# Attention with two heads side by side in column groups of TensorE, the rotary part of the keys on GpSimd

## The chip, the cores and the metric

The kernel runs on one core of a Trainium2 chip. The metric is the device time of one execution in microseconds. TensorE (PE) multiplies, VectorE (DVE) and ScalarE (ACT) work element by element and can read PSUM, GpSimd (POOL) works on SBUF alone, SyncE (SP) issues the DMAs. Each engine runs its own list of instructions in order; semaphores hold one back until another has done its part.

## The reference

Attention over 4 batches of 8 heads, 576 positions of 64 values, with rotary position encoding of queries and keys, then two feed-forward layers of 512 to 2048 to 512.

```python
q_rot, k_rot = rotate(q), rotate(k)          # x1*cos - x2*sin, x1*sin + x2*cos
scores = 1/sqrt(64) * q_rot @ k_rot.T
scores = scores - max(scores, axis=-1)
attn = exp(scores); attn = attn / (sum(attn) + 1e-09)
x = (attn @ v)                               # to [2304 tokens, 512]
h = x @ w_in;   x = (h - tanh(h)) @ w_out          # layer 1
h = x @ w_in2;  x = (h * sigmoid(1.702*h)) @ w_out2  # layer 2
```

## The kernel before

Attention comes first, then the two layers; the layers (`first_product`, `second_product`, `unit`) are not touched by the change. Numbers that need more than fp32r's precision are kept as a high part and a rest, both fp32r: `k_hl` holds the keys' high part in one half of the partitions and the rest in the other, `q_hh` the queries' high part twice, `q_max` the queries' rest and the rows for the maxima, `k_one` the keys' high part and ones.

32 heads are 16 pairs; the keys of a head are five tiles of 128 (the last of 64). For one head PE does, for each of five tiles:
- near scores M(h, t), line 414: queries by keys, two fp32r matmuls of 288 columns, from which DVE takes the row maxima (`row_max`, line 667);
- after five of them one transpose of the maxima (`maxima_across`, line 421), which DVE copies behind the queries (`place_maxima`, line 674);
- scores S(h, t), lines 431 and 437: keys by queries with the maximum taken off in the product, four fp32r matmuls; ACT makes exp of them (`exp`, line 537, into `probs`, five buffers);
- values, `probs_v`, line 449: two fp32 matmuls of 288 columns. The stationary operand `v_one` is 128 wide: 64 columns of V and 64 of ones, so one product gives both values and sums of a head. PSUM banks 6 and 7 hold the result of one head; ACT copies it out (`copy_pv`, line 545).

The six PSUM banks before are a ring of three slots, used in the order of `RING`, S, M and R (the transpose) alike: PE may write a slot when the use three places back has been read (`slot_free`). The order in a head is S, PV of two tiles back, and M tiles of the next head behind the first two S; it is written out in `ring_order` and again in PE's loop. The transpose stands between the third S and the fourth, so it has two more tiles of its head to cover it.

DVE also does the rotary part, `rope`: three operations of 128x576 for the keys of a pair and three for the queries (lines 659 to 662), one or the other in each head, and the rests (`keys_lo` line 679, `queries_lo` line 684). ACT makes the high parts (`keys_hi`, `queries_hi`). SyncE loads, makes the second copies in `k_one` and `q_hh` by DMA, and carries the sums: from `pv_sb` to `sums`, inverted by DVE (`invert`), through DRAM to all partitions (`inv_wide`). GpSimd multiplies (`normalise`, line 382, two operations of 64x576 a pair) and SyncE stores the result. In heads 17 to 31 the x chunks and weights of the first layer are split ahead of time (`early_x`, `early_w`), in DVE's and ACT's lists.

## Time and profile before

| what | us |
|---|---|
| runs | 1146.66, 1146.83, 1147.7; median 1146.83 |
| the profiled execution | 1147.27 |
| its span, first to last instruction | 1145.5 |
| PE busy | 1104.1 (96%) |
| DVE busy | 552.4 (48%) |
| ACT busy | 425.7 (37%) |
| POOL busy | 57.1 (5%) |

TensorE's granted clock is 0.997 of 2.4 GHz over the span. Busy time of PE counts records that overlap: a record of a matmul lasts longer than it takes the next one to start, since the pipeline is long, so the pace is read from the starts. A fp32 matmul of the program is two records with a weight load each; a fp32r one is one record. The shares are means over attention and the layers, which have different limits.

### The profile page before, as it was taken

To read this page: it belongs to the slowest core of one execution; us is meant where nothing else is said; L and a number is where in the kernel's file an instruction comes from. 1 tells how busy PE (TensorE), PEld (TensorE's weight loads), DVE (VectorE), ACT (ScalarE), POOL (GpSimd) and SP (SyncE) were. 2 spreads that over 40 slices of the span, in tenths; PEclk is the share of its full clock that TensorE was granted. 3 is DMA by queue.
4 is the path that set the end of the run, shared out by engine and by line. 5 is a ranking of instruction groups with operands and counts; after the bars stand their busy time and mean duration, and the time that the engine had idled before them with its cause. 6 is when DMAs were issued, how large, how long until landed. Compare 5 with 4: busy or idle time off the path is not lost.

```text
span 1145.5 us, 15078 instructions
## 1 busy us (share of the span) xinstructions
PE 1104.1 (96%) x5952; PEld 1017.8 (89%) x5952; DVE 552.4 (48%) x879; ACT 425.7 (37%) x747; POOL 57.1 (5%) x62
## 2 busy tenths in 40 slices
PE   2999998999999999999999999999999999999998
PEld 1888877787789999999999999999999999999997
DVE  7888887888736433232233333455232322323222
ACT  2555554555544423222222323445232222323222
POOL 3011111102111000000000000000000000000000
PEclk9999999999999999999999999999999999999999
DMA  6355557566315300000000100062000000000000
GB/s 182 95 158 127 155 154 201 136 169 166 87 61 178 102 28 29 28 28 11 19 28 28 29 28 28 1 193 83 28 28 28 28 1 28 28 28 1 28 1 28
DMA packets 78854, 79.85 MB, mean 70 GB/s; under 512 B 30144, under 2 KB 55744, under 8 KB 78784
## 3 DMA queue, kind: packets, MB, share of 16 engines
q1 hardware_dynamic: 78784, 78.89, 24.1%
q8 instruction: 47, 0.77, 0.3%
q14 instruction: 23, 0.19, 0.1%
HBM read 55.12 MB, written 14.23 MB: 61 GB/s over the span
## 4 chain that ended last, share of the span: by engine, by line
PE 89%; DVE 7%; SPq 1%; DMA 1%; POOL 1%; issue 1%; ACT 0%; POOLq 0%; DVEq 0%; ACTq 0%
PE PS L485 35%; PE PS L503 17%; PE PS L500 17%; PE PS L449 10%; PE PS L414 3%; PE PS L431 3%; PE PS L437 3%; DVE neg_max L667 2%; DVE q_max L684 1%; DVE k_hl L679 1%; DVE q_max L674 1%; DMA turned_k<-k_dram 1%; DVE raw_q L662 0%; DVE w_parts L697 0%; DVE raw_q L660 0%
## 5 line engine op out<-in xcount | busy, mean ns | idle before, releaser
L485 PE MATMUL PS<-x_hi,w_parts 128*128 128x384 f32 x1536 | 423.1, 336 | 0.0
L742 DVE TENSOR_TENSOR g_raw<-PS,act_t 128x384 f32<-128x384 f32 x192 | 107.0, 557 | 400.2 <-ACT act_t L610 202.1
L485 PEld LDWEIGHTS PS<-x_hi,w_parts 128*128 128x128 f32 x1536 | 280.5, 188 | 4.3
L485 PE MATMUL PS<-x_lo,w_parts 128*128 128x384 f32 x768 | 257.2, 335 | 0.0
L500 PE MATMUL PS<-g_hi,w_parts 128*128 128x384 f32 x768 | 210.3, 334 | 0.8 <-DVE g_lo L747 0.8
L503 PE MATMUL PS<-w_parts,g_hi 128*128 128x512 f32 x576 | 195.1, 393 | 1.0 <-DVE y_sb L756 0.8
L449 PE MATMUL PS<-probs,v_one 128*128 128x288 f32 x640 | 183.4, 409 | 0.3 <-ACT pv_sb L545 0.3
L747 DVE TENSOR_TENSOR g_lo<-g_raw,g_hi 128x384 fp32r<-128x384 f32 x192 | 107.7, 561 | 113.6 <-ACT g_hi L617 113.6
L537 ACT ACTIVATE probs<-PS 128x576 f32<-128x576 f32 x160 | 104.0, 650 | 129.6 <-PE PS L437 126.3
L485 PEld LDWEIGHTS PS<-x_lo,w_parts 128*128 128x128 f32 x768 | 144.2, 188 | 4.2
L617 ACT ACTIVATE g_hi<-g_raw 128x384 fp32r<-128x384 f32 x192 | 100.8, 525 | 122.9 <-DVE g_raw L742 119.7
L500 PEld LDWEIGHTS PS<-g_hi,w_parts 128*128 128x128 f32 x768 | 140.0, 188 | 1.1 <-DVE g_lo L747 1.1
L449 PEld LDWEIGHTS PS<-probs,v_one 128*128 128x128 f32 x640 | 112.4, 191 | 18.1 <-issue 0.5
L667 DVE TENSOR_REDUCE neg_max<-PS 128x1 f32<-128x576 f32 x160 | 113.8, 746 | 30.1 <-PE PS L414 29.5
L500 PE MATMUL PS<-g_lo,w_parts 128*128 128x384 f32 x384 | 128.3, 334 | 0.0
L503 PEld LDWEIGHTS PS<-w_parts,g_hi 128*128 128x128 f32 x576 | 108.1, 188 | 21.9 <-issue 1.1
L610 ACT ACTIVATE act_t<-PS 128x384 f32<-128x384 f32 x96 | 47.2, 492 | 212.5 <-PE PS L485 212.5
L608 ACT ACTIVATE act_t<-PS 128x384 f32<-128x384 f32 x96 | 47.2, 492 | 206.9 <-PE PS L485 206.9
L414 PE MATMUL PS<-k_hl,q_hh 128*128 128x288 f32 x320 | 86.7, 376 | 34.8 <-DMA q_hh<-q_hh 17.5
L503 PE MATMUL PS<-w_parts,g_lo 128*128 128x512 f32 x288 | 113.7, 395 | 0.0
L414 PEld LDWEIGHTS PS<-k_hl,q_hh 128*128 128x128 f32 x320 | 56.4, 200 | 51.8 <-issue 19.7
L431 PE MATMUL PS<-q_hh,k_hl 128*128 128x288 f32 x320 | 80.0, 332 | 0.0
(51 smaller groups left out, 741.3 us busy)
## 6 DMA issues: line engine op xcount, KB each, us to landing
x_raw<-x_scratch SPq DMA_DIRECT2D x12, 768.0 KB, 4.5
raw_w<-moe_w_in_dram SPq DMA_DIRECT2D x32, 256.0 KB, 3.1
raw_w<-moe_w_out_dram SPq DMA_DIRECT2D x32, 256.0 KB, 3.3
raw_k<-k_dram SPq DMA_DIRECT2D x16, 288.0 KB, 3.5
turned_k<-k_dram SPq DMA_DIRECT2D x64, 72.0 KB, 3.2
raw_q<-q_dram SPq DMA_DIRECT2D x16, 288.0 KB, 3.8
turned_q<-q_dram SPq DMA_DIRECT2D x64, 72.0 KB, 3.5
k_one<-k_hl SPq DMA_DIRECT2D x32, 144.0 KB, 2.4
```

Source lines behind the costliest of these rows:

```text
L414: last = nc.tensor.matmul(slot[:, b, :], q_hh[h % 4][:, t * P:(t + 1) * P], k_hl[h % 4][:, b * HALF:(b + 1) * HALF], start=True, stop=True)
L431: nc.tensor.matmul(slot[:, b, :], k_hl[h % 4][:, keys], q_hh[h % 4][:, b * HALF:(b + 1) * HALF], start=True, stop=False)
L449: last = nc.tensor.matmul(pv_banks[:, b, :], v_one[h // 2 % 2][:, h % 2, t, :], probs[g % PROBS][:, b * HALF:(b + 1) * HALF], start=t == 0 ...
L485: last = nc.tensor.matmul(h_banks[j % 2], w_parts[j][:, w, c * P:(c + 1) * P], x[par][:, c, :], start=(c == 0 and w == 0 and x is x_hi), s ...
L500: last = nc.tensor.matmul(acc_banks[c][:, 0:UNIT], w_parts[j][:, w, c * P:(c + 1) * P], g[:, s, :], start=start, stop=stop)
L503: last = nc.tensor.matmul(acc_banks[c], g[:, s, c * P:(c + 1) * P], w_parts[j][:, w, :], start=start, stop=stop)
L537: nc.scalar.activation(probs[g % PROBS][:, :].rearrange("p (b n) -> p b n", b=2), slot_halves(slot_of("S", h, t)), ACT.Exp).then_inc(exp_d ...
L608: nc.scalar.activation(act_t[:, j % 2, :], h_banks[j % 2], ACT.Tanh).then_inc(act_done, 1)
L617: nc.scalar.activation(g_hi[:, j % STAGES, :], g_raw[:, j % 2, :], ACT.Copy).then_inc(g_hi_done, 1)
L667: nc.vector.tensor_reduce(neg_max[h % 2][:, t:t + 1], slot_halves(slot_of("M", h, t)), AX.XY, ALU.max, negate=True).then_inc(max_done, 1)
L742: nc.vector.tensor_tensor(g_raw[:, j % 2, :], h_banks[j % 2], act_t[:, j % 2, :], ALU.subtract if m == 0 else ALU.mult).then_inc(g_done, 1)
L747: nc.vector.tensor_tensor(g_lo[:, j % STAGES, :], g_raw[:, j % 2, :], g_hi[:, j % STAGES, :].bitcast(F32), ALU.subtract).then_inc(g_lo_don ...
```

## The change

The loops go by pairs, and each step does tile n of both heads.

- `values(unit)` replaces `probs_v`. V of both heads lies in one tile, `v_sb` (laid out so by the host's `value_tiles`); head 0's 64 columns of it go to columns 0 to 63 of the array and PSUM partitions 0 to 63, head 1's to the other half, in matmuls of 512 and of 64 columns. The sums are four matmuls of 288 columns by 32 ones, one for each half of each head, in four groups of 32 columns. Eight fp32 matmuls (sixteen records) replace four (eight).
- `copy_pv` is once a pair: three copies of 512, 64 and 288 columns. The result is one tile of 128x576, normalised in place in one GpSimd operation.
- The rotary part of the keys from pair 1 on is three GpSimd operations a pair; DVE keeps the queries, and both of pair 0.
- The maxima of a pair go out together: two transposes in one slot, in the last step, and the order of M tiles follows `near_plan`. Before the first S all ten M tiles of pair 0 are done.
- Six sets of `k_hl`, `k_one`, `q_hh`, `q_max` instead of four, six `probs` instead of five, some of them in memory that the layers use later.
- The early weights and x stand in pairs 8 to 15.

In the diff the first `rope` is GpSimd's, the last loop over pairs is DVE's, and `split` is `keys_lo` and `queries_lo` of one head.

```diff
+def near_plan(pair):
+    if pair == 0:
+        return [(0, 0), (0, 2), (2, 2), (2, 2), (0, 0)]
+    return [(1, 2), (1, 2), (1, 1), (1, 1), (0, 0)]
...
+        values_wide, values_tail, sum_rows = PS[:, 6, :], PS[:, 7, 0:TAIL], PS[:, 7, TAIL:TAIL + HALF]
...
-            for j in range(4):
+            for j in range(SETS):
                 nc.gpsimd.memset(k_one[j][:, :].bitcast(F32), 0.0)
...
+            def rope(pair):
+                par = pair % 2
+                pool.wait_ge(loaded["k"][par], (pair // 2 + 1) * 80)
+                nc.gpsimd.tensor_tensor(turned["k"][par][:, :], turned["k"][par][:, :], sin_sb[:, :], ALU.mult).then_inc(pool_chain, 1)
+                nc.gpsimd.tensor_tensor(raw["k"][par][:, :], raw["k"][par][:, :], cos_sb[:, :], ALU.mult).then_inc(pool_chain, 1)
+                pool.wait_ge(pool_chain, 3 + 2 * pair)
+                nc.gpsimd.tensor_tensor(raw["k"][par][:, :], raw["k"][par][:, :], turned["k"][par][:, :],
+                                        ALU.add).then_inc(k_roped, 1)
...
+            for pair in range(PAIRS):
                 if pair >= 2:
+                    normalise(pair - 2)
+                if pair + 3 < PAIRS:
+                    rope(pair + 3)
...
-            def probs_v(g):
-                h, t = divmod(g, TILES)
-                pe.wait_ge(exp_done, g + 1)
+            def values(unit):
+                pair, t = divmod(unit, TILES)
+                pe.wait_ge(exp_done, 2 * unit + 2)
                 if t == 0:
-                    pe.wait_ge(loaded["v"][h // 2 % 2], h // 4 * 64 + 64)
-                    if h:
-                        pe.wait_ge(pv_copied, h)
-                for b in range(2):
-                    last = nc.tensor.matmul(pv_banks[:, b, :], v_one[h // 2 % 2][:, h % 2, t, :],
-                                            probs[g % PROBS][:, b * HALF:(b + 1) * HALF], start=t == 0, stop=t == TILES - 1)
-                last.then_inc(pv_done, 1)
+                    pe.wait_ge(loaded["v"][pair % 2], pair // 2 * 16 + 16)
+                    if pair:
+                        pe.wait_ge(pv_copied, pair)
+                first, last = t == 0, t == TILES - 1
+                p = [probs[(2 * unit + a) % PROBS] for a in range(2)]
+                for bank, cols in ((values_wide, slice(0, BANK)), (values_tail, slice(BANK, SEQ))):
+                    for a in range(2):
+                        nc.tensor.matmul(bank[own(a), :], v_sb[pair % 2][:, t, own(a)], p[a][:, cols],
+                                         start=first, stop=last, skip_group_check=True)
+                for g in range(4):
+                    done = nc.tensor.matmul(sum_rows[32 * g:32 * g + 32, :], ones[:, t // FULL, :],
+                                            p[g // 2][:, g % 2 * HALF:(g % 2 + 1) * HALF], start=False, stop=last,
+                                            skip_group_check=True)
+                done.then_inc(pv_done, 1)
...
+            for h, t in near_tiles(0):
+                near_scores(h, t)
+            maxima_across(0)
+            for pair in range(PAIRS):
+                for n, (first, second) in enumerate(pair_steps(pair)):
+                    scores(2 * pair, n)
+                    for h, t in first:
+                        near_scores(h, t)
+                    if pair * TILES + n:
+                        values(pair * TILES + n - 1)
+                    if n == TILES - 1 and pair + 1 < PAIRS:
+                        maxima_across(pair + 1)
+                    scores(2 * pair + 1, n)
+                    for h, t in second:
+                        near_scores(h, t)
...
+            def copy_pv(pair):
+                act.wait_ge(pv_done, (pair + 1) * TILES)
+                if pair >= 3:
+                    act.wait_ge(x_stored[(pair - 3) % 2], (pair - 3) // 2 * 16 + 16)
+                nc.scalar.activation(pv_sb[pair % 3][:, 0:BANK], values_wide, ACT.Copy)
+                nc.scalar.activation(pv_sb[pair % 3][:, BANK:SEQ], values_tail, ACT.Copy)
+                if pair >= 2:
+                    act.wait_ge(sums_in[pair % 2], pair // 2 * 64)
+                nc.scalar.activation(sum_sb[pair % 2][:, :], sum_rows, ACT.Copy).then_inc(pv_copied, 1)
...
+            for pair in range(PAIRS):
+                a, b = 2 * pair + 4, 2 * pair + 5
+                for n, (first, second) in enumerate(pair_steps(pair)):
...
+                    for h, t in first + second:
+                        row_max(h, t)
+                    if pair and b < NHEADS and n == 1:
+                        split(a)
+                    if pair and b < NHEADS and n == 3:
+                        split(b)
+                    if n == 3 and pair:
+                        invert(pair - 1)
+                    if n == TILES - 1 and pair + 1 < PAIRS:
+                        for h in (2 * pair + 2, 2 * pair + 3):
+                            place_maxima(h)
...
+                    if n == TILES - 1 and pair + 3 < PAIRS:
+                        rope(pair + 3)
```

PE's list in the first half of a head in the steady part, before. L431 and L437 are S, L449 is PV of one head, L414 is M of the next head.

```order
L431 MATMUL PS<-q_hh,k_hl 128x288 x2
L437 MATMUL PS<-q_max,k_one 128x288 x2
L449 MATMUL PS<-probs,v_one 128x288 x2
L414 MATMUL PS<-k_hl,q_hh 128x288 x4
L431 MATMUL PS<-q_hh,k_hl 128x288 x2
L437 MATMUL PS<-q_max,k_one 128x288 x2
L449 MATMUL PS<-probs,v_one 128x288 x2
L421 MATMUL PS<-ident,neg_max 5x128
L431 MATMUL PS<-q_hh,k_hl 128x288 x2
```

PE's list in one step of a pair and the start of the next, now. L466 and L472 are S, L447 is M, L488 the values of both heads, L492 the four sums.

```order
L466 MATMUL PS<-q_hh,k_hl 128x288 x2
L472 MATMUL PS<-q_max,k_one 128x288 x2
L447 MATMUL PS<-k_hl,q_hh 128x288 x2
L488 MATMUL PS<-probs,v_sb 64x512 x2
L488 MATMUL PS<-probs,v_sb 64x64 x2
L492 MATMUL PS<-probs,ones 32x288 x4
L466 MATMUL PS<-q_hh,k_hl 128x288 x2
L472 MATMUL PS<-q_max,k_one 128x288 x2
L447 MATMUL PS<-k_hl,q_hh 128x288 x4
L466 MATMUL PS<-q_hh,k_hl 128x288 x2
L472 MATMUL PS<-q_max,k_one 128x288 x2
L447 MATMUL PS<-k_hl,q_hh 128x288 x2
```

The work on values stands in one block a step, between the two heads' scores, instead of one behind each S.

DVE's list for one head before (L667 is a row maximum, L659 to L662 the rotary part, L674 the placing of the maxima, L679 and L684 the rests):

```order
L667 TENSOR_REDUCE neg_max<-PS 128x1 x5
L659 TENSOR_TENSOR turned_k<-turned_k,sin_sb 128x576
L660 TENSOR_TENSOR raw_k<-raw_k,cos_sb 128x576
L662 TENSOR_TENSOR raw_k<-raw_k,turned_k 128x576
L674 TENSOR_TENSOR q_max<-PS,g_raw 5x640
L679 TENSOR_TENSOR k_hl<-raw_k,k_hl 64x576
L684 SCALAR_TENSOR_TENSOR q_max<-raw_q,q_hh 64x576
```

DVE's list for one pair now (L743 is a row maximum, L755 and L760 the rests, L767 and L769 the inverse, L750 the placing, L736 to L739 the rotary part of the queries):

```order
L743 TENSOR_REDUCE neg_max<-PS 128x1 x6
L755 TENSOR_TENSOR k_hl<-raw_k,k_hl 64x576
L760 SCALAR_TENSOR_TENSOR q_max<-raw_q,q_hh 64x576
L743 TENSOR_REDUCE neg_max<-PS 128x1 x4
L755 TENSOR_TENSOR k_hl<-raw_k,k_hl 64x576
L760 SCALAR_TENSOR_TENSOR q_max<-raw_q,q_hh 64x576
L767 TENSOR_SCALAR sums<-sums 128x9
L769 RECIPROCAL sums<-sums 128x9
L750 TENSOR_TENSOR q_max<-PS,g_raw 5x640 x2
L736 TENSOR_TENSOR turned_q<-turned_q,sin_sb 128x576
L737 TENSOR_TENSOR raw_q<-raw_q,cos_sb 128x576
L739 TENSOR_TENSOR raw_q<-raw_q,turned_q 128x576
```

Both placings stand together at the end of a pair, behind the rests of the second head, with the rotary part behind them; three operations of the keys are gone.

## Rows read from the trace of the kernel before

**Rows 1.** The page: span, and busy time of each engine (share) xinstructions
```profile
span 1145.5 us, 15078 instructions
...
PE 1104.1 (96%) x5952; PEld 1017.8 (89%) x5952; DVE 552.4 (48%) x879; ACT 425.7 (37%) x747; POOL 57.1 (5%) x62
```

**Rows 2.** Sums by stretch: length, busy time by engine, clock, DMA share, GB/s
```profile
100.90:119.10 18.20, 18.16 (x105) 15.51 (x104) 16.00 (x25) 10.44 (x17) 2.81 (x2) 1.00 0.57 149
155.50:319.60 164.10, 151.16 (x819) 126.59 (x818) 136.60 (x194) 86.91 (x135) 26.91 (x18) 0.98 0.56 147
319.60:340.30 20.70, 20.39 (x112) 17.54 (x110) 5.94 (x9) 8.65 (x13) 4.21 (x3) 1.00 0.17 55
340.30:1145.50 805.20, 800.11 (x4309) 761.11 (x4307) 279.00 (x480) 252.59 (x481) 3.07 (x2) 1.00 0.12 39
```

**Rows 3.** Timeline, first scores of pairs 0, 2, 15: start, us, engine, line
```profile
23.82 0.68 PE L431 MATMUL PS<-q_hh,k_hl 128*128 128x288 f32 x2
...
64.50 0.42 PE L431 MATMUL PS<-q_hh,k_hl 128*128 128x288 f32 x2
...
319.57 0.42 PE L431 MATMUL PS<-q_hh,k_hl 128*128 128x288 f32 x2
```

**Rows 4.** Timeline of PE in a steady pair, its PV groups
```profile
114.75 1.15 PE L449 MATMUL PS<-probs,v_one 128*128 128x288 f32 x4
...
116.37 1.13 PE L449 MATMUL PS<-probs,v_one 128*128 128x288 f32 x4
...
117.86 1.13 PE L449 MATMUL PS<-probs,v_one 128*128 128x288 f32 x4
...
119.62 1.13 PE L449 MATMUL PS<-probs,v_one 128*128 128x288 f32 x4
```

**Rows 5.** Timeline, scores handed to ScalarE
```profile
200.46 0.43 PE L437 MATMUL PS<-q_max,k_one 69*128 69x288 f32 x2
...
200.93 0.65 ACT L537 ACTIVATE probs<-PS 128x576 f32<-128x576 f32 x1 [0.55 <-PE PS L437]
```

**Rows 6.** Timeline, ScalarE copies and makes exp, GpSimd beside, PE after
```profile
331.46 0.65 ACT L545 ACTIVATE pv_sb<-PS 128x576 f32<-128x576 f32 x1 [0.32 <-PE PS L449]
...
331.85 1.40 POOL L382 TENSOR_TENSOR x_out<-pv_sb,inv_wide 64x576 f32<-64x576 f32 x1 [10.84 <-DMA inv_wide<-inv_scratch]
332.01 0.65 ACT L537 ACTIVATE probs<-PS 128x576 f32<-128x576 f32 x1
...
332.26 0.72 PE L449 MATMUL PS<-probs,v_one 128*128 128x288 f32 x2 [0.31 <-ACT pv_sb L545]
```

**Rows 7.** Instructions by line and form: busy us, mean ns of one, idle before
```profile
L667 DVE TENSOR_REDUCE neg_max<-PS 128x1 f32<-128x576 f32 x160 | 113.8, 746 | 30.1 <-PE PS L414 29.5
...
L537 ACT ACTIVATE probs<-PS 128x576 f32<-128x576 f32 x160 | 104.0, 650 | 129.6 <-PE PS L437 126.3
...
L382 POOL TENSOR_TENSOR x_out<-pv_sb,inv_wide 64x576 f32<-64x576 f32 x32 | 48.3, 1508 | 298.0 <-DMA inv_wide<-inv_scratch 246.4 <-issue 50.7
...
L674 DVE TENSOR_TENSOR q_max<-PS,g_raw 5x640 fp32r<-5x640 f32 x32 | 25.9, 811 | 2.9 <-PE PS L421 2.5
...
L625 ACT ACTIVATE y_sb<-PS 128x512 f32<-128x512 f32 x10 | 5.4, 596 | 2.2 <-PE PS L503 2.2
L625 ACT ACTIVATE y_sb<-PS 128x384 f32<-128x384 f32 x12 | 5.2, 488 | 2.2 <-PE PS L500 2.2
```

**Rows 8.** Timeline, a split of VectorE beside GpSimd's product
```profile
185.80 1.68 POOL L382 TENSOR_TENSOR x_out<-pv_sb,inv_wide 64x576 f32<-64x576 f32 x1 [21.05 <-issue]
186.24 1.87 DVE L684 SCALAR_TENSOR_TENSOR q_max<-raw_q,q_hh 64x576 fp32r<-64x576 f32 x1
```

**Rows 9.** Timeline of the start: GpSimd's fourth set, VectorE's first rotary operation
```profile
8.07 0.14 POOL L369 MEMSET q_hh<- 128x64 f32 x1
...
9.90 0.70 DVE L659 TENSOR_TENSOR turned_k<-turned_k,sin_sb 128x576 f32<-128x576 f32 x1
```

**Rows 10.** Who waited for whom on PE in attention: us, times, longest
```profile
PE PS L414 <- DVE neg_max L667: 12.6, 9, 3.1
```

420 lines of the change are left out of this document (218 added, 202 removed).

## The prediction, made before the changed kernel ran

> **What bounds the kernel now.** I read the page's busy times first, then the sums by stretch, then one pair of heads in the timeline, then the waits. The page shows TensorE (PE) busy for 96% of 1145.5 us [rows 1]. The stretches say which part the change can touch: from 340.3 us on PE only runs the two layers, whose code is the same in both kernels, so 805 us are fixed. Attention, 0 to 340 us, has four pieces [rows 2, 3]: a start up to the first scores of pair 2 (64.5 us); five steady pairs, 18.2 us each, with PE busy 18.16 of 18.20 us in the one shown; eight pairs from 155.5 to 319.6 us, 20.5 us each, with PE busy 151 of 164 us; and a last pair of 20.7 us, of which 2.1 us are twelve fp32r matmuls of the first layer (384 columns at the pace of 0.27 us for two of 288, below), so 18.6 us are attention. In the eight slow pairs PE's near scores wait for row maxima, 12.6 us over all of attention [rows 10]: VectorE (DVE) has the weight and x splits of the early layer in its queue there, and it is busy 16.0 of 18.2 us even in a steady pair [rows 2].
>
> The pair in parts [rows 4]. From one PV group to the next is 1.49 us where scores alone stand between them (116.37 to 117.86); two fp32r matmuls (one near-score tile, M) add 0.27 (117.86 to 119.62); the transpose of the maxima adds 0.13 (114.75 to 116.37). A fp32 matmul is two records, each with a weight load of its own; four records last 1.13 us and the last of them 0.41, so one pass of 288 columns takes (1.13 - 0.41) / 3 = 0.24 us, and one head's PV tile four passes = 0.96. A score tile (S) is then 1.49 - 0.96 = 0.53. A pair is 10 S + 10 M + 2 transposes + 10 PV = 5.3 + 2.7 + 0.26 + 9.6 = 17.9 us of the 18.2: PE is the bound, with 0.3 us of waiting.
>
> **What the change does to PE.** One call of `values` replaces two PV tiles. By columns, a pass of 512 is 0.24 x 512 / 288 = 0.43 us and one of 64 is 0.05. If the column groups work beside each other, the unit costs 2 x 0.43 (both heads' first 512 columns) + 2 x 0.05 + 2 x 0.24 (the four sums) = 1.44; I take 1.5 for sixteen starts instead of eight. The pair falls to 5.3 + 2.7 + 0.26 + 5 x 1.5 = 15.8 us of PE work, 2.1 less. No row of the kernel before has a matmul with fewer than 128 columns of weights, but for the transpose, so the bounds of a unit are 1.44 below and, above, all sixteen passes in a row: 4 x 0.43 + 4 x 0.05 + 8 x 0.24 = 3.84, twice the 1.92 of now. I take the lower end because the 0.24 is the streaming of columns and the groups stream apart.
>
> **New waits.** PE's order is new, and it runs in order through a ring of three slots; a wait there delays all that follows. Handing over costs 0.20 us from the end of streaming to ScalarE (ACT): the record of the last scores ends at 200.89, 0.16 after its stream, and exp starts at 200.93 [rows 5]. Back to PE it costs 0.15 (ACT's copy ends 332.11, PE's row starts 332.26 [rows 6]). With exp 0.65, row maximum 0.74, place 0.81 [rows 7] and the fact that DVE starts an operation about 0.07 before the last one's record ends, one pair has:
> - The maxima of both heads go out together. The first of the two transposes to the first `place_maxima` done and back is 0.20 + 0.81 + 0.15 = 1.16; PE has the second transpose, S of the second head and half an S meanwhile, 0.13 + 0.53 + 0.27 = 0.93. Wait 0.25 to 0.3.
> - The next pair's first M takes the slot of the transposes and waits for the second place, 0.74 later, with 0.27 of scores to cover it: 0.45.
> - M tiles of step 0 wait for the first row maximum, queued behind three rotary operations of the queries (3 x 0.70 [rows 9]): 0.25.
> - Step 1's first S takes the slot of the second head's S of step 0. Its exp stands behind `copy_pv`, now three copies. Copies of 512 and 384 columns take 0.596 and 0.488 [rows 7], so 64 takes 0.22 and 288 takes 0.41; each starts 0.1 before the last ends (332.01 against 332.11 [rows 6]), 0.9 in all. From the end of `values`: 0.20 + 0.9 + 0.65 + 0.15 = 1.9, against S + 2 M + the wait above = 1.3 on PE: 0.6.
> - Step 2's first S waits for the exp of the second head's S of step 1: 0.20 + 0.65 + 0.15 = 1.0 against 2 M = 0.53: 0.45.
> - Step 3's first S waits for a row maximum that stands behind the splits of the next head (`split(a)`): 0.2, and 0.8 when a split collides with GpSimd (below).
> - The last unit waits for the exp just before it: 1.0 - 0.27 - 0.53 = 0.2.
>
> That is 2.4 to 3.1 us. The new pair is 15.8 + 2.4 = 18.2, to 15.8 + 3.1 = 18.9; I take 18.6. So the 2.1 us won on PE are given back as waits at handovers, because PE's work between them has become shorter while the exp, maxima and copies have not.
>
> **Rotary part on GpSimd.** It takes three operations of 128x576 per pair from DVE (2.1 us of DVE's 16.0) and gives them to GpSimd, where one of 64x576 costs 1.51 mean, 1.4 alone [rows 6, 7]; more lanes at the same column count should cost the same. GpSimd goes from 2 operations to 4 a pair, 2.8 to 5.6 us. When a DVE operation with two operands in SBUF meets one of these it stands until it is through: the split at 186.24 takes 1.87 instead of 0.75, ending 0.6 after GpSimd's operation of 185.80 does [rows 8]. Row maxima, which read PSUM, are not held. GpSimd's block of four (5.6 us, from inv_wide's arrival on) meets `split(a)` in most pairs; none met costs 0, one met up to 1.4 on DVE, of which 0.6 reaches PE by the item above. The Trainium skill (SBUF — State Buffer, "SBUF: two separate sides") calls the shared port pair an exclusive lock, held for the whole instruction; the trace agrees with its 1.87 us.
>
> **Start.** GpSimd clears six sets, not four: four sets end at 8.21 [rows 9], having begun at 2.88, so two more at 1.33 us each end at 10.9, while the clears of v_one behind them go. DVE's first rotary operation moves from 9.90 [rows 9] to 11.3. Before the first S there are ten row maxima instead of five (+3.4 us), and the splits of the second head ahead of them (+1.5), less the 3 rotary operations of keys that stood there (-2.2): first S near 27 against 23.8, near 30 if GpSimd's keys of pair 1 meet DVE's first rotary operations. Pairs 0 and 1 then run by DVE's list (9 rotary operations, 12 splits, 20 maxima, 4 places: 6.3 + 8.4 + 13.5 + 3.0 = 31 us, and some 10 us of waiting for first exps and copies), about 41.5 us against 40.7. Pair 2 starts at 68 to 73; I take 70.
>
> **The slow pairs.** DVE's list is three operations shorter, so a weight split (two per head pair at most) fits: DVE has 13.9 + 1.2 = 15.1, with a collision 16.5, of 18.6. I leave no dent there. This is the only place of real gain.
>
> **Sum** against the profiled execution (1147.3 us, its span 1145.5 and 1.8 around it): start 70 - 64.5 = +5.5; thirteen pairs 13 x 18.6 = 241.8 against 319.6 - 64.5 = 255.1, -13.3; last pair 5.3 + 7.5 + waits where no M covers (5 or so of about 1 us) = 18.1 against 18.6, -0.5. Together -8.3: 1139.0. The median of the runs is 0.4 below the profiled execution, so 1138.6, and I say 1139. SyncE issues about as many DMAs a pair as before (23 against 24) and hides them; at the end of attention the inverse of the last pair has several units to travel, as before.
>
> **Rivals.**
> 1. *The waits are shorter than laid out.* For: the ring may run further ahead than my handovers allow. Then a pair is 15.8 + 0.9 = 16.7, thirteen are 38 us shorter, start +3.5, last pair -2: -36.5, 1110 us. Against: seven handovers of 0.2 and more are all in the rows.
> 2. *The array drains when the column tiling changes.* A record outlasts its streaming by 0.41 - 0.24 = 0.16 us [rows 4]; three changes a unit (whole array to halves to quarters and back) make it 1.5 + 0.48 = 1.98. Eighty units are 38 us, of which about 6 are waits that PE has anyway: 1139 + 32 = 1171 us. The transpose, the one narrow matmul of now, shows no such cost (0.13 us for 128 columns). The Trainium skill (TensorEngine Tiling (Array Packing), "Tiling Modes") says that changing the mode drains the engine; no run here shows it yet.
> 3. *The other side, in one mechanism: passes start strictly in order.* In `values` both passes of one matmul stand together. The second waits for the first on the same columns, and the other head's first pass behind it. Then only neighbours overlap: 3 x 0.43 + 2 x 0.05 + 5 x 0.24 = about 2.55 a unit, 1.05 more; 80 x 1.05 = 84, of which about 19 cover waits that PE has anyway (row maxima and splits have more time): 1139 + 65 = 1204 us. For: PE's records start in order everywhere. It decides as soon as a unit is over 1.6 us, since each 0.1 us is 8 us of kernel. The Trainium skill (TensorE: Matmul & The Clock Gate, "Part 3: Packing small matmuls — row/col tiling") has matmuls in strict order in start and end; that would give this case.
> 4. *The groups don't overlap at all.* 3.84 a unit, 80 x 2.34 = 187 less the same 19: 1139 + 168 = 1307 us. The change doesn't do what it says then.
>
> **Chances.** Forecast (overlap and waits as laid out, 1126 to 1150) 0.50; rival 1 0.18; rival 2 0.13; rival 3 0.11; rival 4 0.06; 0.02 for others. A run of this kernel can be told from no change at about 0.2%, 2.3 us. Faster: 0.18 + 0.50 x 0.72 = 0.54. Same: 0.08. Slower: 0.06 of the forecast's own tail and rivals 2 to 4 and the rest: 0.38. The range 1104 to 1185 takes in the forecast, rival 2 and most of rival 1, and leaves out 3 and 4 and the far end of 1, just under 0.2.
>
> **What would show it.** Right: from one unit of `values` to its end 1.5 us; starts of two column groups together; pairs of 18.2 to 18.9 us with PE's idle time at the first S of steps 1, 2 and 3 and behind q_max; rotary operations on GpSimd with DVE splits of 1.5 to 2.2 us beside them; pair 2 at about 70 us; the layers as long as before. Wrong: a unit of over 1.6 us (rivals 2 to 4), a pair under 17.5 (rival 1), or pairs 8 to 15 longer than pairs 2 to 7.

## The result, and the profile after

The changed kernel takes 1188.24 us (median of 4 runs, 1183.38 to 1191.1), the kernel before 1146.74 beside it: ratio 1.0356, 95% interval 1.032 to 1.0392. It is 3.6% slower, 49 us above the forecast. The profiled execution took 1187.16 us.

The page of the kernel after (compare [rows 1]); parts 1, 2 and 4:

```profile
span 1185.4 us, 16265 instructions
PE 1118.9 (94%) x6592; PEld 953.3 (80%) x6592; DVE 540.2 (46%) x835; ACT 418.1 (35%) x763; POOL 109.0 (9%) x93
PEclk9899999999999999999999999999999999999999
PE 82%; DVE 13%; ACT 2%; issue 2%; POOL 1%; DMA 1%; SPq 0%; POOLq 0%; DVEq 0%; ACTq 0%
```

PE is still most of the chain that ended last. Its busy sum is 15 us above that of [rows 1] although fewer columns are streamed, and the span grew by 40. The stretches say where. They are cut at the first scores of pairs 0, 2, 7 and 15 (length, busy time by engine, granted clock, DMA share, GB/s):

```profile
0.00:31.06 31.06, 6.34 (x22) 4.54 (x23) 20.89 (x29) 4.10 (x6) 19.26 (x38) 0.99 0.59 163
31.06:77.74 46.68, 41.15 (x271) 24.67 (x269) 34.22 (x48) 20.80 (x34) 8.40 (x6) 0.89 0.39 103
77.74:183.63 105.89, 95.41 (x712) 57.87 (x711) 77.79 (x106) 49.63 (x85) 33.10 (x20) 1.00 0.50 129
183.63:357.82 174.19, 155.70 (x1139) 93.62 (x1137) 126.11 (x170) 81.98 (x140) 43.32 (x26) 0.98 0.50 137
357.82:1185.40 827.58, 820.28 (x4458) 772.58 (x4456) 281.23 (x485) 261.57 (x498) 4.93 (x3) 1.00 0.12 40
```

Against [rows 2, 3]: up to pair 2 77.7 us for 64.5 (+13.2); five pairs 105.9 for 91.0 (+14.9); eight pairs 174.2 for 164.1 (+10.1); from pair 15 to the end 827.6 for 825.9 (+1.7). That is the 39.9.

**One unit of values.** PE, and below it PE's weight loads, of one unit in pair 4 (L447 M, L488 the values, L492 the sums, L466 the next S):

```profile
122.28 0.53 PE L447 MATMUL PS<-g_hi,g_lo 128*128 128x288 f32 x2 [0.25 <-DVE q_max L750]
122.74 0.64 PE L488 MATMUL PS<-probs,v_sb 128*64 128x512 f32 x1
122.74 0.64 PE L488 MATMUL PS<-y_sb,v_sb 128*64 128x512 f32 x1
123.22 0.59 PE L488 MATMUL PS<-probs,v_sb 128*64 128x512 f32 x1
123.22 0.59 PE L488 MATMUL PS<-y_sb,v_sb 128*64 128x512 f32 x1
123.64 0.22 PE L488 MATMUL PS<-probs,v_sb 128*64 128x64 f32 x1
123.65 0.22 PE L488 MATMUL PS<-y_sb,v_sb 128*64 128x64 f32 x1
...
123.86 0.44 PE L492 MATMUL PS<-probs,ones 128*32 128x288 f32 x2
123.87 0.44 PE L492 MATMUL PS<-y_sb,ones 128*32 128x288 f32 x2
124.13 0.41 PE L492 MATMUL PS<-probs,ones 128*32 128x288 f32 x2
...
124.48 0.53 PE L466 MATMUL PS<-q_hh,k_hl 128*128 128x288 f32 x2
```
```profile
122.73 0.13 PEld L488 LDWEIGHTS PS<-probs,v_sb 128*64 128x64 f32 x1 [0.16 <-ACT y_sb L580]
...
124.48 0.30 PEld L466 LDWEIGHTS PS<-q_hh,k_hl 128*128 128x128 f32 x2 [0.47 <-issue]
```

The two heads start together (122.74), their second passes together (123.22), the four sums together (123.86): the column groups overlap wholly. The gaps are elsewhere. A record ends 0.16 after its stream, so M's streaming ends at 122.28 + 0.53 - 0.16 = 122.65; the first weights of the tiled matmuls go in at 122.73 and their stream starts at about 122.79 (the second pass at 123.22 less its 0.43), 0.14 later. The tails' stream ends at 123.76 and the sums start at about 123.88: 0.12. The sums' second pass streams to 124.38, and only at 124.48 does the weight load of the next S begin (between matmuls of the whole array it lies under the streaming before it), so S streams from about 124.58: 0.20. Three changes of tiling, 0.46 us a unit on top of 1.48 of streaming. The starts of streams are worked out from rows and good to some 0.02 us.

The whole unit from rows of pair 5, where nothing is waited for:

```profile
156.90 1.19 PE L488 MATMUL PS<-probs,v_sb 128*64 128x512 f32 x8
158.03 0.69 PE L492 MATMUL PS<-probs,ones 128*32 128x288 f32 x8
158.65 0.53 PE L466 MATMUL PS<-g_lo,g_hi 128*128 128x288 f32 x2
...
160.19 0.64 PE L488 MATMUL PS<-probs,v_sb 128*64 128x512 f32 x1
```

From unit to unit 3.29 us, with two S and one M between (2 x 0.53 + 0.27 = 1.33): a unit is 1.96 us. Two PV tiles before were 1.92 [rows 4]. The quarter of the columns that the change saves is spent on the changes of tiling.

**The waits.** PE in pair 5, its rows with idle time ahead of them (in brackets):

```profile
142.55 0.50 PE L472 MATMUL PS<-q_max,k_one 69*128 69x288 f32 x2 [0.41 <-DVE q_max L750]
143.30 0.53 PE L447 MATMUL PS<-k_hl,q_hh 128*128 128x288 f32 x2 [0.25 <-DVE q_max L750]
...
147.26 0.53 PE L466 MATMUL PS<-g_lo,g_hi 128*128 128x288 f32 x2 [0.42 <-ACT y_sb L580]
...
151.53 0.54 PE L466 MATMUL PS<-g_lo,g_hi 128*128 128x288 f32 x2 [0.21 <-ACT y_sb L580]
...
155.91 0.53 PE L466 MATMUL PS<-g_lo,g_hi 128*128 128x288 f32 x2 [0.58 <-DVE neg_max L743]
```

These are five of the seven places that the prediction lists, with the releasers it names. The brackets miss the 0.16 by which a record outlasts its stream; with it the five are 2.7 us. For the other two places no row shows idle time. The pair lasts 21.0 us and its work is 5.3 + 2.7 + 0.26 + 5 x 1.96 = 18.1, so 2.9 us are waits. The last of the five is the collision. VectorE, then GpSimd, in front of it:

```profile
153.33 1.85 DVE L760 SCALAR_TENSOR_TENSOR q_max<-raw_q,q_hh 64x576 fp32r<-64x576 f32 x1
155.11 1.40 DVE L743 TENSOR_REDUCE neg_max<-PS 128x1 f32<-128x576 f32 x2
```
```profile
152.64 1.93 POOL L401 TENSOR_TENSOR turned_k<-turned_k,sin_sb 128x576 f32<-128x576 f32 x1
154.54 1.92 POOL L402 TENSOR_TENSOR raw_k<-raw_k,cos_sb 128x576 f32<-128x576 f32 x1
156.54 1.41 POOL L404 TENSOR_TENSOR raw_k<-raw_k,turned_k 128x576 f32<-128x576 f32 x1
```

Alone a 128x576 operation takes 1.41 us on GpSimd, as 64x576 did. When they meet, both records get longer (1.93 and 1.85), and the ends show that they take turns: GpSimd's first ends at 154.57, VectorE's split 0.61 later (155.18), GpSimd's second 1.28 after that (156.46). Each stands until the other's operation is through.

**The start.** VectorE's rotary part of the first queries, and beside it GpSimd's of pair 1:

```profile
13.55 1.96 DVE L728 TENSOR_TENSOR turned_q<-turned_q,sin_sb 128x576 f32<-128x576 f32 x1
15.43 1.95 DVE L729 TENSOR_TENSOR raw_q<-raw_q,cos_sb 128x576 f32<-128x576 f32 x1
17.41 1.83 DVE L731 TENSOR_TENSOR raw_q<-raw_q,turned_q 128x576 f32<-128x576 f32 x1
```
```profile
13.42 1.47 POOL L401 TENSOR_TENSOR turned_k<-turned_k,sin_sb 128x576 f32<-128x576 f32 x1 [2.56 <-DMA turned_k<-k_dram]
14.86 1.91 POOL L402 TENSOR_TENSOR raw_k<-raw_k,cos_sb 128x576 f32<-128x576 f32 x1
16.84 1.79 POOL L404 TENSOR_TENSOR raw_k<-raw_k,turned_k 128x576 f32<-128x576 f32 x1
```

VectorE's three take 5.7 us, 3.5 more than at 0.75, and all that follows stands behind them: first M at 22.5, first S at 31.1.

**The clock.** The mean granted clock was 1.00 in eleven of the pairs from 2 to 14 and 0.93 in pairs 8 and 10, so for a part of those two at the lower of its two levels, 1.2 GHz. Those two took 23.6 and 23.4 us from first exponential to first exponential; the other six of pairs 7 to 14 took 21.1 on average, as much as a steady pair. The kernel before has two such pairs too, 8 and 14, with 24.4 and 22.4 us.

### The profile page after: what moved, and what is told of

Same layout as the page of the kernel before. It is cut to its first block, busy times and chain, and to the rows that moved or that the text cites. A ratio compares the mean times of both kernels' runs of the same rounds, so it can differ in the third digit from the quotient of the medians.

```text
span 1185.4 us, 16265 instructions
## 1 busy us (share of the span) xinstructions
PE 1118.9 (94%) x6592; PEld 953.3 (80%) x6592; DVE 540.2 (46%) x835; ACT 418.1 (35%) x763; POOL 109.0 (9%) x93
## 4 chain that ended last, share of the span: by engine, by line
PE 82%; DVE 13%; ACT 2%; issue 2%; POOL 1%; DMA 1%; SPq 0%; POOLq 0%; DVEq 0%; ACTq 0%
PE PS L529 33%; PE PS L547 17%; PE PS L544 17%; PE PS L488 5%; DVE neg_max L743 4%; PE PS L492 3%; PE PS L466 3%; DVE q_max L760 3%; PE PS L447 2%; DVE q_max L750 2%; PE PS L472 2%; DVE k_hl L755 1%; ACT y_sb L580 1%; DVE g_hi L755 1%; ACT probs L580 0%
## 5 line engine op out<-in xcount | busy, mean ns | idle before, releaser
L743 DVE TENSOR_REDUCE neg_max<-PS 128x1 f32<-128x576 f32 x160 | 116.0, 752 | 82.2 <-PE PS L447 82.0
L580 ACT ACTIVATE y_sb<-PS 128x576 f32<-128x576 f32 x79 | 51.4, 652 | 90.7 <-PE PS L472 90.4
L580 ACT ACTIVATE probs<-PS 128x576 f32<-128x576 f32 x81 | 52.5, 650 | 71.2 <-PE PS L472 70.9
L472 PE MATMUL PS<-q_max,k_one 69*128 69x288 f32 (+1 forms) x320 | 70.4, 302 | 5.9 <-DVE q_max L750 5.7
L447 PE MATMUL PS<-k_hl,q_hh 128*128 128x288 f32 x220 | 47.8, 317 | 28.3 <-DMA q_hh<-q_hh 22.9
L544 PEld LDWEIGHTS PS<-g_lo,w_parts 128*128 128x128 f32 x384 | 72.1, 188 | 0.0
L488 PE MATMUL PS<-probs,v_sb 128*64 128x512 f32 (+1 forms) x324 | 67.9, 438 | 0.8 <-ACT probs L580 0.6
```

Source lines behind the costliest of these rows:

```text
L447: last = nc.tensor.matmul(slot[:, b, :], q_hh[h % SETS][:, t * P:(t + 1) * P], k_hl[h % SETS][:, b * HALF:(b + 1) * HALF], start=True, sto ...
L472: last = nc.tensor.matmul(slot[:, b, :], k_one[h % SETS][rows, keys], q_max[h % SETS][rows, b * HALF:(b + 1) * HALF], start=False, stop=True)
L488: nc.tensor.matmul(bank[own(a), :], v_sb[pair % 2][:, t, own(a)], p[a][:, cols], start=first, stop=last, skip_group_check=True)
L544: last = nc.tensor.matmul(acc_banks[c][:, 0:UNIT], w_parts[j][:, w, c * P:(c + 1) * P], g[:, s, :], start=start, stop=stop)
L580: nc.scalar.activation(probs[i % PROBS].rearrange("p (b n) -> p b n", b=2), slot_halves(slot_of("S", h, t)), ACT.Exp).then_inc(exp_done, 1)
L743: nc.vector.tensor_reduce(neg_max[h % 2][:, t:t + 1], slot_halves(slot_of("M", h, t)), AX.XY, ALU.max, negate=True).then_inc(max_done, 1)
```

## The experiments

Three theories, of which more than one can hold. A: the changes of tiling eat what the columns save. B: PE's new order of work waits more. C: GpSimd's rotary part blocks VectorE. (The expectations of single runs have letters of their own; their ranges are called first, second and third below.) Pair starts are read at the first exponential of a pair. Every kernel in a row, in us (the time is the median, the parts are of the profiled execution; the last column has the pairs of 2 to 14 whose mean granted clock was below 0.99):

| kernel | time | to pair 2 | pairs 2 to 6 | pairs 7 to 14 | lower clock |
|---|---|---|---|---|---|
| before | 1146.7 to 1148.4 | 65.2 | 91.0 | 164.1 | 8, 14 |
| changed | 1188.2 | 79.1 | 105.9 | 173.9 | 8, 10 |
| whole-array values | 1191.6 | 79.2 | 109.7 | 174.2 | 12 |
| four changes a unit | 1195.5 | 80.2 | 109.6 | 173.5 | none |
| sums in the last unit only | 1170.5 | 77.9 | 105.5 | 161.1 | 2, 3, 8, 9, 14 |
| keys on VectorE | 1207.9 | 84.6 | 112.5 | 184.3 | 3, 5, 6, 8, 10 to 13 |
| before, PV in two groups | 1178.7 | 71.3 | 105.7 | 171.6 | none |
| before, keys on GpSimd | 1174.2 | 72.4 | 96.3 | 172.9 | 8, 13 |
| two units together | 1167.9 | 89.1 | 96.6 | 159.2 | none |
| other places of M | 1177.0 | 80.0 | 102.3 | 167.4 | 7 |
| two units, start anew | 1160.6 | 76.7 | 96.8 | 159.9 | none |
| copies behind, in addition | 1156.8 | 73.2 | 98.0 | 159.9 | none |
| start anew alone | 1185.8 | 76.2 | 110.1 | 171.8 | 2 |
| start again | 1156.2 | 69.0 | 98.4 | 160.8 | none |

The last column is needed to read the others: a pair at the lower clock is longer by its clock alone (in "keys on VectorE" below, by 1.5 us).

### Whole-array values in the changed kernel

```diff
-(the two loops of values and the four sums)
+for a in range(2):
+    for b in range(2):
+        matmul(wide[b], v_sb[pair % 2][:, t, :], p[a][:, b * HALF:(b + 1) * HALF], ...)
```

> The values and sums of a unit are replaced by four fp32 matmuls of 288 columns on the whole array (128 columns of weights), as in the kernel before: V of both heads as the weights for each head's exp, sums left out, the result is not attention's. Everything else (order, copies, GpSimd's rotary part, waits) is the changed kernel. Theory A (the tiled unit costs 1.94 us with three drains of 0.12 to 0.20 at changes of tiling, just what 1.92 us of whole-array matmuls cost; the 40 us come from the new order's waits and start): 1183 to 1191 us, no change against the changed kernel. Theory B (narrow matmuls are what costs the time): falls to about 1150 us.

Measured: 1191.58 us (1188.91 to 1192.54), ratio 1.0376 (1.0359 to 1.0394). With no tiling at all and the old columns, the time is within 4 us of the changed kernel, 0.6 above the first range and far from the second one's 1150. A tiled unit is worth as much as an untiled one; and the 40 us are still there, so they belong to the order and the start.

### A fourth change of tiling

```diff
-values wide, values tail, sums
+values tail, sums, values wide
```

> Same matmuls, other order inside a unit: the 64-column tail of both heads, then the four sums, then the 512 columns of both heads. The tiling changes four times a unit (whole, halves, quarters, halves, whole) instead of three. Theory A (a change drains the array, 0.12 to 0.20 us by the trace): +0.12 to 0.2 us on 80 units, 10 to 16 us, so 1197 to 1204 us. Theory C (the gaps in the trace come from waits or exposed weight loads at the group's ends and not from changes of tiling): 1186 to 1190 us.

Measured: 1195.48 (1192.26 to 1198.18), ratio 1.0413 (1.0389 to 1.0437). 7 us for 80 more changes, 0.09 each: between the two ranges, in the direction of the first. By itself this shows little, since pairs 2 to 6 also take 109.7 and 110.1 us in two kernels that have no more changes than the changed one (the table); that part of a change falls into waits is a reading, not shown.

### Sums only in the last unit of a pair

```diff
-for g in range(4):
+for g in range(4) if last else ():
```

> The four sum matmuls run only in the last unit of a pair (left out: the sums over the first four key tiles). In 64 of 80 units 0.48 us of streaming and one change (0.12) go. Theory A (PE's work and its waits are in one chain): 64 x 0.6 = 38 us less, of which waits fill a part: 1150 to 1162 us. Theory D (VectorE's list or handovers are the bound in attention and PE merely waits): under 10 us less, 1178 to 1187.

Measured: 1170.51 (1169.1 to 1177.63), ratio 1.0214 (1.0176 to 1.0252), 18 us less, between the two ranges. What leaves PE is 64 times a sum (0.48) and a change (0.12), 38 us. Half of it turned into waits. Pairs 2, 3 and 5 (the last three numbers of a row: granted clock, DMA share, GB/s):

```profile
77.90:99.80 21.90, 18.12 (x110) 11.77 (x110) 15.98 (x22) 9.92 (x17) 6.58 (x4) 0.92 0.45 124
99.80:123.30 23.50, 19.68 (x111) 12.38 (x110) 16.25 (x22) 10.02 (x17) 6.47 (x4) 0.85 0.45 116
143.10:163.50 20.40, 16.58 (x110) 10.93 (x110) 16.02 (x22) 9.91 (x17) 6.59 (x4) 1.00 0.49 133
```

The five together take 105.5 for 105.9, but pairs 2 and 3 ran partly at the lower clock. Pairs 4 to 6, at full clock in both kernels, take 60.0 us for 62.9: 2.9 less of the 7.2 that left PE. The rest are longer waits at the same places. In pair 5 PE stands 1.92 us where it stood 0.58, and 1.04 where it stood 0.41:

```profile
156.02 0.52 PE L466 MATMUL PS<-g_lo,g_hi 128*128 128x288 f32 x2 [1.92 <-DVE neg_max L743]
163.00 0.50 PE L472 MATMUL PS<-q_max,k_one 69*128 69x288 f32 x2 [1.04 <-DVE q_max L750]
```

That is B: the pair is set in part by the chain from scores over row maxima and placed maxima back to PE, and not by PE's work alone. It is also the forecast's own case. The five units of a pair are here 4 x 1.36 + 1.96 = 7.4 us, 1.5 each, as forecast, and the pair takes 20.0 us at full clock, not 18.6.

### Keys' rotary part back on VectorE

```diff
-nc.gpsimd.tensor_tensor(...)   # three a pair
+nc.vector.tensor_tensor(...)   # ahead of those of the queries
```

> The rotary part of all keys goes back to VectorE, directly ahead of that of the queries; GpSimd only normalises. Theory A (the order of PE's work and what it waits for is the loss, GpSimd's lock a minor part): VectorE gets 2.1 us a pair more in the place where the first row maximum of a pair waits for it, loses 1 to 2 us of blocked splits: 1180 to 1200 us. Theory E (GpSimd's operations blocking VectorE are the loss): falls by 20 us or more, 1150 to 1165.

Measured: 1207.93 (1207.43 to 1209.77), ratio 1.0525 (1.051 to 1.0541): 20 us slower and above both ranges. C falls as the main cause: without the collisions a pair at full clock is no shorter (21.6 us for 21.4). In this order VectorE does its rotary part right behind the placed maxima, and the first row maxima of a pair stand behind it. PE's waits for row maxima show it (us, times, longest; changed kernel first):

```profile
PE PS L466 <- DVE neg_max L743: 11.3, 11, 1.7
```
```profile
PE PS L441 <- DVE neg_max L738: 27.7, 14, 4.0
```

Part of the 20 us is the clock. Of pairs 2 to 10 the four at full clock took 21.6 us each, against 21.4 for the same four in the changed kernel, and the five at 0.93 took 23.1. PE falls to half its pace behind the 1.66 us that it stands for a row maximum (a record of 0.64 before is 1.12 here):

```profile
156.04 0.53 PE L441 MATMUL PS<-k_hl,q_hh 128*128 128x288 f32 x2 [1.66 <-DVE neg_max L738]
157.53 1.12 PE L482 MATMUL PS<-probs,v_sb 128*64 128x512 f32 x1
```

Pair 4 has the same wait and stays at 1.00, so not each such wait brings it. What the six operations cost by their place alone is therefore less than the 20 us, and no run gives it at one clock.

### The kernel before, its PV in two column groups

```diff
 for b in range(2):
-    matmul(pv_banks[:, b, :], v_one[..., t, :], probs[...])
+    for a in range(2):
+        matmul(pv_banks[own(a), b, :], v_one[..., t, own(a)], probs[...])
```

> The kernel before, with one edit: each values matmul of a head (128 stationary columns, 288 moving columns) is issued as two, one for each half of its stationary columns, side by side in two column groups of 64. Same operands, same output, same order, same everything else; only the tiling of the array changes, twice in each of the 160 head-units (from whole to two groups before values, and back after). Theory A (the array drains at every change of tiling: 0.14 us into it and 0.20 us out of it in the trace of the changed kernel, and the matmul stream is what bounds the kernel before): 160 x 0.34 = 54 us more, less what falls into waits that are there anyway in the slow pairs: 1185 to 1202. Theory B (a change of tiling costs nothing, and the changed kernel's time went to its order of work alone): within 5 us of the kernel before, 1142 to 1152. Theory C (only the weight loads of the tiled matmuls stand still, some 0.07 a change): 1160 to 1172.

Measured: 1178.67 (1177.44 to 1178.73), ratio 1.026 (1.0244 to 1.0275). 30.5 us slower with the same columns, order and results. The sum over one steady pair ([rows 2] have it at 18.20 us, PE 18.16, 105 PE rows):

```profile
113.60:134.70 21.10, 21.10 (x144) 13.11 (x146) 16.12 (x25) 10.43 (x16) 2.82 (x2) 1.00 0.48 127
```

2.9 us for ten PV tiles with two changes each: 0.145 us a change where PE is the bound. It is not the doubled number of matmuls: the eight records of a tile last 1.19 us together, 0.06 more than the four before (1.13 [rows 4]), and the other 0.23 of the 0.29 lies at the two edges. In pairs 7 to 14, which have waits, only 7.5 of 23 us come through (some 3 more, by estimate, if the two pairs of the kernel before at the lower clock are set aside), and so the total is under the 54 of the first range. The time lies in none of the three ranges; B alone (no more than 5 us) is out: a change of tiling costs by itself.

### The kernel before, keys' rotary part on GpSimd

```diff
-rope("kq"[h % 2], h // 2 + 2)        # VectorE
+if h % 2: rope("q", h // 2 + 2)      # VectorE
+rope(pair + 2)                       # GpSimd, keys, ahead of normalise
```

> The kernel before, with one part of the change: from the second pair on GpSimd does the rotary part of the keys (three operations of 128x576 a pair), VectorE that of the queries alone. If VectorE's row maxima are what the eight slow pairs of the kernel before wait for, taking 2.2 us of it a pair away gives back part of the 18.5 us by which these pairs are longer than 18.2 each: 1133 to 1145. If the collision of GpSimd and VectorE (1.8 us for an operation of 0.75) falls on row maxima and splits of the tight pairs, it costs up to 1 us a pair: 1147 to 1160; and the start is longer by 2 to 5 us in either case, since GpSimd's first rotary part lies beside VectorE's. I take 1144.

Measured: 1174.17 (1168.58 to 1180.98), ratio 1.0226 (1.0183 to 1.0269). I had expected 1144, and it is above the other range too. VectorE, then GpSimd, in a steady pair:

```profile
129.69 1.77 DVE L704 SCALAR_TENSOR_TENSOR q_max<-raw_q,q_hh 64x576 fp32r<-64x576 f32 x1
```
```profile
129.03 1.82 POOL L391 TENSOR_TENSOR turned_k<-turned_k,sin_sb 128x576 f32<-128x576 f32 x1 [11.10 <-DMA turned_k<-k_dram]
```

The keys' operations now meet VectorE's splits, and the row maximum behind them comes 0.8 us late: 19.3 us a pair for 18.2. PE's waits for row maxima rise from 12.6 us [rows 10] to 27.5. So the collision alone is worth 1.1 us a pair where nothing else waits, and C holds as a part: to move work to GpSimd costs here about half of what it frees on VectorE. Of the profiled execution's excess 7.2 us are in the start, 5.3 in pairs 2 to 6 and 8.8 in pairs 7 to 14. It is the fastest of the four; the others took 1173.58, 1174.75 and 1180.98 us at a mean clock of 0.991, 0.990 and 0.988 for its 0.995.

### Two units of values together

```diff
-values(pair * TILES + n - 1)                       # every step
+if n == 0: values([prev]);  if n in (2, 4): values([two units])
-    return [(1, 2), (1, 2), (1, 1), (1, 1), (0, 0)]
+    return [(2, 1), (1, 1), (2, 1), (1, 1), (0, 0)]
```

> The changed kernel, with values of two units back to back (wide and tail of both, then the sums of both) at the third and the fifth step of a pair, so that a pair has 9 changes of tiling in place of 15, and 3, 2, 3, 2 of the next pair's near scores in its steps (2 and 1, 1 and 1, 2 and 1, 1 and 1). Theory A (a change costs 0.12 to 0.20 us, 6 fewer a pair): 0.9 us less a pair, 14 in all, and with fewer waits at steps without values up to 1 us a pair more: 1160 to 1175. If the waits take it all back: 1183 to 1192. If the steps without values starve the matmul stream: above 1195.

Measured: 1167.91 (1167.1 to 1171.08), ratio 1.0174 (1.0154 to 1.0194), 20 us less. A double unit:

```profile
134.59 1.19 PE L488 MATMUL PS<-y_sb,v_sb 128*64 128x512 f32 x8
...
136.69 0.69 PE L495 MATMUL PS<-y_sb,ones 128*32 128x288 f32 x8
...
137.79 0.53 PE L466 MATMUL PS<-q_hh,k_hl 128*128 128x288 f32 x2
```

3.20 us from its first row to the first of S, against 1.74 for a single one (122.74 to 124.48); with the 0.2 that lies outside these rows 3.4 against 3.9. Two doubles a pair save 1.0. A pair fell from 21.0 to 19.2, and the other 0.8 us are waits that the new places of M took away. Pairs 0 and 1 became 10 us longer: without values in their first steps PE stands longer for the copies of the next heads, which come late there (12.1 us of waits from 31 us to pair 2, for 7.3). Beside it the clock was lower for longer (some 21 us after 36 us, for some 5), and the two are not told apart.

### Only other places of M

```diff
-    return [(1, 2), (1, 2), (1, 1), (1, 1), (0, 0)]
+    return [(0, 1), (2, 1), (2, 1), (2, 1), (0, 0)]
```

> The changed kernel, with only the places of the next pair's near scores changed: none in the first step before the unit of values and one behind it, then two before and one behind in the three steps that follow. Theory A (half of the loss is waits of the order, not work): the order of the near scores alone moves the time: at the pair's start the first unit of values no longer stands behind a near score that waits for the second head's placed maxima, 0.5 to 1 us less a pair: 1172 to 1181. If the waits only move: 1185 to 1191. If three near scores in a step are more than VectorE's row maxima keep up with: 1195 to 1205.

Measured: 1176.96 (1174.56 to 1178.31), ratio 1.0242 (1.0219 to 1.0264). The same instructions, in another order of ten of PE's near scores a pair, give 11 us, inside the first range: B is shown by itself.

### The start laid out anew, with the double units and alone

```diff
+pool.wait_ge(q_lo_done, 2)            # ahead of GpSimd's first rope
-for j in range(SETS): (pads)          # VectorE, ahead of the first rope
+set_pads((0, 1)); rope_first(k, q); set_pads((2, 3, 4, 5))
+rope(1)                               # VectorE, ahead of the first row maxima
```

> Both together: values of two units back to back with that run's places of the near scores, and the start laid out anew: GpSimd's first rotary part waits until VectorE has split the first pair's heads, two of the six sets of padding are set before the first rotary part, VectorE rotates the queries of the second pair before the first row maxima and those of the third pair in the first pair's second step, ScalarE makes the high parts of the first four heads before the first exponential. If the 13.2 us which the start costs over the kernel before are such waits, and a matmul stream at half clock behind them, the two effects add: 15 to 22 us less than 1167.9, 1146 to 1153. If the stream fills the start anyway (the half clock of the first 20 us stays, whatever waits are gone): 1159 to 1165.

Measured: 1160.59 (1159.6 to 1163.26), ratio 1.0111 (1.0091 to 1.013). This lies in the second range.

> The changed kernel with the start laid out anew alone (as in the first run of this list), its pairs as they were. The start is 77.7 us to the third pair in the changed kernel and 64.5 in the kernel before. If the order of the first 60 us is what costs it: 7 to 12 us less than 1188.2, 1176 to 1181. If it is the unit of values and the waits of the pairs that also fill the first two pairs: 2 to 5 us less, 1183 to 1186.

Measured: 1185.77 (1184.59 to 1187.98), ratio 1.0327 (1.0304 to 1.0351). Alone it brings 2.4 us, in the second range, but the runs of the two kernels overlap (1183.4 to 1191.1 against 1184.6 to 1188.0), so that is not told from nothing. In the trace 2.9 go up to pair 2, and then pairs 2 to 6 are 4.2 longer, of which 2.2 are pair 2 at a clock of 0.93, and pairs 7 to 14 are 2.1 shorter. With the double units it brings 7, mostly what those had lost in pairs 0 and 1. Pads and GpSimd's first block were only moved onto VectorE's next operations there (in the trace of the next kernel, whose start is the same, two operations of rope(1) take 1.97 and 1.84 us, and PE waits 3.8 us for a row maximum).

### Copies behind both exponentials, and the start once more

```diff
 exp(2 * pair, n)
-if n == 0 and pair: copy_pv(pair - 1)
 exp(2 * pair + 1, n)
+if n == 0 and pair: copy_pv(pair - 1)
...
-    return [(2, 1), (1, 1), (2, 1), (1, 1), (0, 0)]
+    return [(2, 2), (0, 1), (2, 1), (1, 1), (0, 0)]
```

> The kernel of the run before in this list, with ScalarE's copies of the sums of products (1.2 us a pair) behind both first exponentials of a pair in place of between them, and 4, 1, 3, 2 near scores in a pair's steps in place of 3, 2, 3, 2. If the score that waits 0.2 us for an exponential behind the copies is what is left of the waits of a pair: 0.2 to 0.4 us less a pair, 3 to 5 us less. If the two waits of 0.2 us that the trace shows in a pair only move: within 2 us of that run.

Measured: 1156.8 (1155.83 to 1159.23), ratio 1.0077 (1.0058 to 1.0096). 3.8 us less as forecast, but from the time up to pair 2 (3.5), not from the steady pairs (98.0 for 96.8): the number was right and its reason wrong. In those two pairs the clock went down twice in the run before it (at 47 and 61 us) and here not again once it was up, so the 3.5 can be the clock.

```diff
-pool.wait_ge(q_lo_done, 2)
+pool.wait_ge(q_roped, 1)              # GpSimd's first rope, later
-set_pads((2, 3, 4, 5))                # VectorE
+for j in range(2, SETS): nc.gpsimd.memset(k_one[j][max_rows(j % 2), 0:SEQ], 1.0)
...
-    return [(2, 2), (0, 1), (2, 1), (1, 1), (0, 0)]
+    return [(2, 1), (1, 1), (2, 1), (1, 1), (0, 0)]
```

> The kernel with the copies behind both exponentials, with three more edits: GpSimd sets the padding of the last four pairs' sets itself while it is idle (2.8 us of VectorE ahead of the first splits go), GpSimd's first rotary part waits until VectorE has rotated the queries of the second pair (two operations of 1.97 and 1.84 us in place of 0.75, and a wait of 3.8 us of the matmul stream behind them), and 3, 2, 3, 2 near scores in a pair's steps in place of 4, 1, 3, 2 (19.2 us a pair in place of 19.5). Start 3 to 4 us less, five pairs up to 1 us less: 1151 to 1154, still above the kernel before. If the collision in the start only moves to the first row maxima and splits: 1155 to 1158. Below 1146.7 only if the start ends as early as that of the kernel before.

Measured: 1156.21 (1154.38 to 1160.01), ratio 1.008 (1.0061 to 1.0099). VectorE, then GpSimd, in its start:

```profile
16.13 0.75 DVE L743 TENSOR_TENSOR raw_q<-raw_q,cos_sb 128x576 f32<-128x576 f32 x1
```
```profile
17.92 1.40 POOL L408 TENSOR_TENSOR turned_k<-turned_k,sin_sb 128x576 f32<-128x576 f32 x1 [4.57 <-DVE raw_q L745]
```

No operation is stretched, and the first exponential comes at 28.1 us for 27.1 before. The profiled executions differ by 2.9 us, the medians by 0.6: the step is there in the trace and not to be told in the times. The time lies in the second range, though its reason, a collision that only moves, did not come. This order is still 0.8% behind the kernel before. Its pairs take 19.2 to 19.8 us for 18.2; no version tried beats it.

## Why the prediction was wrong

Two steps failed. Both are in the sum for a pair, 15.8 us of work and 2.4 to 3.1 of waits.

- **The unit of `values`, "I take 1.5 for sixteen starts instead of eight".** It measured 1.96. I read from the transpose that a narrow matmul costs nothing extra; but the transpose (128x5) has few columns of weights and does not split the array into groups, so its 0.13 us [rows 4] said nothing on that. The overlap was right, and rivals 3 and 4 are out: the first passes of both heads start at one time, and the second passes too. Rival 2 had the mechanism and the size (1.98). The Trainium skill (TensorEngine Tiling (Array Packing), "Tiling Modes") says that a change of mode drains the engine; by this trace it is 0.12 to 0.20 us, and 0.145 in the kernel before with two groups.
- **The waits as a term that is added to whatever PE does.** The number was right, 2.9 us for 2.4 to 3.1, and so were five of the seven places; that it fits is luck in part, for it was measured behind units of 1.96. In the kernel with sums in the last unit only, with units of 1.5 on average, the work is 15.7 us and the pair 20.0: 4.3 us of waits. The prediction saw that "the 2.1 us won on PE are given back as waits"; it stopped too early. The step-3 wait for a row maximum, taken at 0.2 to 0.8, was 1.2 to 1.9 there, the wait for the first placed maxima, taken at 0.3, was 1.0.
- **What each is worth.** A steady pair took 21.0 us for 18.6. The unit alone is 0.46 x 5 = 2.3, which would explain it by arithmetic; the run says that 1.0 of it comes back when the unit is as forecast, and that the other 1.4 stays. Over thirteen pairs that run has 266.6 us for 279.8 in the changed kernel and 241.8 in the forecast, with five pairs at the lower clock for two. And in the whole, that run of 1170.5 us is the changed kernel at the forecast's unit (with most sums left out): of the 49 us by which the forecast missed, 18 are the unit and 31 are not. Rival 2 let 6 of its 38 us fall into waits; 20 did.
- **The start, 70 us (68 to 73): 77.7.** The three stretched operations of VectorE are 3.5 of the 7.7. The meeting was named ("near 30 if GpSimd's keys of pair 1 meet DVE's first rotary operations") and the lower case taken. Nine units at 0.46 would be 4.1, but eight units of the first two pairs without their sums brought only 1.2 of 4.8, so what the rest of the start is stays open.
- **"I leave no dent" in the slow pairs.** Six of the eight have none: 21.1 us each, as a steady pair. Pairs 8 and 10 took 23.6 and 23.4, at a clock of 0.93 for 1.00; four other kernels with a clock of 1.00 in these pairs and single units, tiled or not, took 20.5 to 22.3. In the kernel before, the prediction put the length of these pairs down to VectorE; but of its 12.6 us of waits 3.1 are in the start, and two of the eight pairs were at the lower clock.
- **GpSimd's 128x576 costs as 64x576: right** (1.41 alone). The collision at 0.6 a pair was too small as a cost of the move, 1.1 where nothing else waits. In the changed order the kernel with the keys on VectorE is 20 us slower, part of it by its clock.
- **The last pair, -0.5: +1.7.** Its units at 0.46 more would be 2.3; no run takes it apart.

Of the 40 us over the kernel before, the unit gives none (1.96 for 1.92), the waits of the pairs 25 (14.9 + 10.1), the start with the collision 13, the last pair the rest. The range ended at 1185 because rival 2 was laid on the forecast's own waits and start.

What stays open: how a change of 0.145 splits between waiting for the stream to run out and loading weights without cover; the 0.20 on the way back to the whole array, where the load begins only at 124.48, suggests the second, and no run separates them. When the clock falls in a pair, and how much of a kernel's loss is that, was not tested by a run. And the five steady pairs vary by 4 us with small shifts of the start; where GpSimd's block falls and the clock of single pairs both change with it, and no run separates these either. Keys on VectorE at another place than right behind the placed maxima was not tried.

## What to carry to other kernels

Price a tiled matmul by its changes of tiling first, about 0.15 us each where PE is the bound: work saved in a group must be several times that, or the tiled matmuls must be put together (two units in a row were worth 1 us a pair). Ask of any such step what stands on both sides of it: the same columns in the old order cost 30 us when tiled. When an order puts two consumers' work in one block, count the handovers on the chain before counting what PE saves, and count them again for the shorter work: here half of what was taken off PE came back as waits. And read the granted clock of each pair before two kernels are compared by a sum over pairs: 105.5 for 105.9 looked like no gain and hid one of 2.9 us in three pairs.
